# Tap softmax of a fused attention and mixture-of-experts kernel: two parts or three

## The reference, cut to what matters

```
# attention: x (2, 3584, 192), weight_gen (2, 3584, 8 heads, 7 taps), fp32
w = weight_gen - max(weight_gen, axis=-1)          # the tap softmax
w = exp(w);  w = w / (sum(w, axis=-1) + 1e-9)
x_pad = [6 zero rows, x]                            # per batch
out[s, h, :] = sum_k w[s, h, k] * x_pad[s + k, h, :]   # head h: 24 columns
# then mixture 1: noisy gate (x @ w_gate, softplus(x @ w_noise) * noise),
#   the best two of 8 experts, relu(x @ w1[e]) @ w2[e], weighted
# then mixture 2: gate by cosine to 8 embeddings, the best expert alone
```

## Time and profile before

| what | value |
| --- | --- |
| median of 3 runs | 1272.02 us (1271.82 to 1272.87) |
| the profiled execution's own time | 1273.49 us |
| its span | 1271.7 us |
| PE busy in the span | 1100.1 us (87%) |
| DVE busy | 791.9 us (62%) |
| POOL busy | 578.8 us (46%) |
| ACT busy | 552.8 us (43%) |
| first tap product starts | 20.75 us |
| product of the last group starts | 108.50 us |

### The profile page before, as it was taken

The page is one execution under the profiler, slowest core; times in us unless marked ns, Lnnn a source line. Parts: engine busy times, 40 slices in busy tenths (PEclk is TensorE's granted clock), DMA queues, the critical chain, the costliest instruction groups (busy, mean ns, idle before and its releaser), DMA issues.

```text
span 1271.7 us, 28030 instructions
## 1 busy us (share of the span) xinstructions
PE 1100.1 (87%) x7950; PEld 1024.6 (81%) x7951; DVE 791.9 (62%) x1447; ACT 552.8 (43%) x1544; POOL 578.8 (46%) x676
## 2 busy tenths in 40 slices
PE   1999045899999999999999999877179999999997
PEld 1566012799999999999999999856059999999997
DVE  8997899445555464645545464466964655466663
ACT  2112165445444454545444454346544544455552
POOL 5778065344444444444444444400544444444444
PEclk9999555899999999999999999988569999999999
DMA  9111200311313131221313111173603313114421
GB/s 319 70 51 62 58 0 0 90 39 42 97 38 93 43 98 37 62 70 41 101 37 89 43 39 40 37 239 110 232 19 95 94 41 96 42 50 131 130 57 36
DMA packets 51158, 97.51 MB, mean 77 GB/s; under 512 B 9651, under 2 KB 33051, under 8 KB 50876
## 3 DMA queue, kind: packets, MB, share of 16 engines
q1 hardware_dynamic: 33084, 61.77, 15.9%
q0 software_dynamic: 18048, 35.42, 9.7%
HBM read 69.62 MB, written 29.10 MB: 78 GB/s over the span
## 4 chain that ended last, share of the span: by engine, by line
PE 74%; DVE 16%; issue 4%; POOL 2%; ACT 1%; DMA 1%; DVEq 1%; ACTq 0%; POOLq 0%; SPq 0%
PE banks L624 21%; PE banks L626 10%; PE banks L610 8%; PE banks L612 7%; PE banks L611 7%; PE banks L616 7%; PE banks L615 7%; DVE prods L874 3%; PE banks L536 2%; DVE lo_hot L974 2%; POOL prods L410 2%; PE banks L595 2%; PE banks L596 2%; DVE hi_eq L967 2%; PE banks L577 1%
## 5 line engine op out<-in xcount | busy, mean ns | idle before, releaser
L1040 DVE SCALAR_TENSOR_TENSOR h_lo<-banks,h_hi 128x256 fp32r<-128x256 f32 x736 | 312.1, 424 | 380.6 <-ACT h_hi L761 377.5
L761 ACT ACTIVATE h_hi<-banks 128x256 fp32r<-128x256 f32 x736 | 282.5, 384 | 462.4 <-PE banks L616 462.2
L624 PE MATMUL banks<-w_hl,h_hi 128*128 128x384 f32 x1472 | 468.6, 355 | 0.6 <-issue 0.6
L626 PE MATMUL banks<-w_hl,h_lo 128*128 128x192 f32 x1472 | 370.7, 252 | 0.0
L626 PEld LDWEIGHTS banks<-w_hl,h_lo 128*128 128x128 f32 x1472 | 279.1, 190 | 0.0
L624 PEld LDWEIGHTS banks<-w_hl,h_hi 128*128 128x128 f32 x1472 | 276.6, 188 | 1.2 <-issue 1.1
L435 POOL DMA_INDIRECT x_slots<-token_rows,gather_idx x192 | 194.2, 1011 | 105.3 <-POOL gather_idx L432 76.0
L610 PE MATMUL banks<-x_hi_a,w_hi 128*128 (+1 forms) x736 | 227.3, 309 | 8.7 <-DVE h_lo L1040 8.6
L611 PE MATMUL banks<-x_hi_a,w_lo 128*128 (+1 forms) x736 | 207.3, 282 | 0.0
L612 PE MATMUL banks<-x_lo_a,w_hi 128*128 (+1 forms) x736 | 206.8, 281 | 0.0
L615 PE MATMUL banks<-x_hl_b,w_hi 128*128 (+1 forms) x736 | 206.0, 280 | 0.0
(11 more groups left out here) (174 smaller groups left out, 1424.9 us busy)
## 6 DMA issues: line engine op xcount, KB each, us to landing
raw<-in_moe_w SPq DMA_DIRECT2D x17, 768.0 KB
choices<-choice_rows SPq DMA_DIRECT2D x28, 384.0 KB, 3.8
raw<-in_moe_w SPq DMA_DIRECT2D x17, 512.0 KB
raw<-in_moe_w SPq DMA_DIRECT2D x34, 256.0 KB
x_halo<-in_x SPq DMA_DIRECT2D x2, 2688.0 KB, 15.4
token_rows<-stage SPq DMA_DIRECT2D x14, 384.0 KB, 2.3
token_rows<-rows SPq DMA_DIRECT2D x14, 384.0 KB, 4.0
x_slots<-token_rows,gather_idx POOLq DMA_INDIRECT x192
```

The lines of the kernel that those rows point to most:

```text
L624: mm(y[:, i, 0:2 * D], h_hi[:, c % HBUFS, t], w2_hl[u][:, c, :, :], start=c == 0, stop=False)
L626: ins = mm(y[:, i, 0:D], h_lo[:, c % HBUFS, t], w2_hl[u][:, c, 0, :], start=False, stop=c == FC - 1)
L761: sc.activation(h_hi[:, c % HBUFS, :], banks[:, c % HBANKS, 0:BLOCK], ACT.Relu).then_inc(h_hi_ready[m], 1)
L1040: v.scalar_tensor_tensor(h_lo[:, c % HBUFS, :], banks[:, c % HBANKS, 0:BLOCK], 0.0, h_hi[:, c % HBUFS, :].bitcast(F32), ALU.max, ALU.subtr ...
```

## The change

The softmax is done in three parts in place of two: part 0 is the first 8 rows of each partition in batch 0 (groups 0 and 1, 448 weights to a partition), part 1 the other 20 rows of batch 0 (groups 2 to 6, 1120 weights), part 2 batch 1 (groups 7 to 13, 1568 weights). SP loads weights and rows part by part, each row load after its own weights, and `emb` after all of them. DVE does subtraction and multiplication of part 0, POOL those of parts 1 and 2. The steps of parts 1 and 2 stand inside the group loop. The core of the diff:

```
+    PARTS = ((0, 0, 2 * GROUP), (0, 2 * GROUP, J), (1, 0, J))
...
@@ SP
+            load_weights(0)
+            load_x(0)          # two halo DMAs, then the rows
+            load_weights(1)
+            load_x(1)          # rows alone
+            load_weights(2)
+            load_x(2)          # two halo DMAs, then the rows
             sp.dma_start(emb_sb[0:E], emb).then_inc(emb_in, 16)
...
@@ POOL
+            def center(i):
+                pool.wait_ge(tap_max, i + 1)
+                gp.tensor_tensor(w, w, red.unsqueeze(2).to_broadcast(w.shape), ALU.subtract).then_inc(centered[i], 1)
+            def scale(i):
+                pool.wait_ge(exps, i + 1)
+                pool.wait_ge(tap_scale, i + 1)
+                gp.tensor_tensor(w, w, total.unsqueeze(2).to_broadcast(w.shape), ALU.mult).then_inc(weights_scaled[i], 1)
+            center(1)
             for g in range(NG):
                 ... three pair additions of group g ...
+                if g == 0:
+                    scale(1)
+                if g == 1:
+                    center(2)
+                if g == 4:
+                    scale(2)
...
@@ ACT
-            for b in range(B):
-                act.wait_ge(centered[b], 1)
-                sc.activation(attn_w[:, b], attn_w[:, b], ACT.Exp).then_inc(exps, 1)
-            act.wait_ge(emb_in, 16)
-            ... Square and sqrt of emb ...
+            exp_weights(0)
             take_weights(0)
             take_weights(1)
+            exp_weights(1)
             take_weights(2)
             take_turned(0, 0)
             for g in range(2, NG):
+                if g == 3:
+                    exp_weights(2)
                 if g + 1 < NG:
                     take_weights(g + 1)
                 take_logits(0, g - 2, 2 * E)
                 take_turned(0, g - 1)
+                if g == 4:
+                    ... wait for emb, Square and sqrt of emb ...
...
@@ DVE
+            taps_max(0)
+            ... subtraction of part 0 ...
+            taps_sum(0)        # sum, + 1e-9, reciprocal
+            ... multiplication of part 0 ...
             for g in range(NG):
+                for i in part_first(g):
+                    dve.wait_ge(x_in[i], 48 if PARTS[i][1] == 0 else 16)
                 ...
                 tap_products(g, 0, FIRST, first_prods)
+                if g == 0:
+                    taps_max(1)
                 tap_products(g, FIRST, SECOND, second_prods)
+                if g == 0:
+                    taps_sum(1)
+                if g == 1:
+                    taps_max(2)
+                if g == 3:
+                    taps_sum(2)
                 if g > 0:
                     dve.wait_ge(second_prods, g)
                     finish_rows(g - 1)
```

More of the change, by code:

```diff
@@ L178, in attention_moe_moe @@
         consts_ready = sem("consts_ready")
-        attn_w_in = [sem(f"attn_w_in{b}") for b in range(B)]
+        attn_w_in = [sem(f"attn_w_in{i}") for i in range(len(PARTS))]
         emb_in = sem("emb_in")
-        x_in = [sem(f"x_in{b}") for b in range(B)]
+        x_in = [sem(f"x_in{i}") for i in range(len(PARTS))]
         halo_zeroed = sem("halo_zeroed")
@@ L190, in attention_moe_moe @@
         emb_ready = sem("emb_ready")
-        centered = [sem(f"centered{b}") for b in range(B)]
+        centered = [sem(f"centered{i}") for i in range(len(PARTS))]
         tap_max = sem("tap_max")
         tap_scale = sem("tap_scale")
-        weights_scaled = [sem(f"weights_scaled{b}") for b in range(B)]
+        weights_scaled = [sem(f"weights_scaled{i}") for i in range(len(PARTS))]
         exps = sem("exps")
@@ L274, in turned_bank, with part_first, weight_part @@
             return 4 - 2 * u * m
+        def part_first(g):
+            b, jj = divmod(g, GB)
+            return [i for i, (at, lo, _) in enumerate(PARTS) if (at, lo) == (b, jj * GROUP)]
+        def weight_part(i):
+            b, lo, hi = PARTS[i]
+            heads = slice(lo * H, hi * H)
+            return attn_w[:, b, heads, :], attn_red[:, b, heads], tap_sum[:, b, heads]
         def logits_bank(m):
@@ L312, in _, with load_weights, load_x @@
             xt = x.rearrange("b (p j) d -> b p j d", p=P)
-            for b in range(B):
-                sp.dma_start(attn_w[:, b], weight_gen[b].rearrange("(p j) h k -> p (j h) k", p=P)).then_inc(attn_w_in[b], 16)
+            def load_weights(i):
+                b, lo, hi = PARTS[i]
+                rows = weight_gen[b].rearrange("(p j) h k -> p (j h) k", p=P)
+                sp.dma_start(weight_part(i)[0], rows[:, lo * H:hi * H, :]).then_inc(attn_w_in[i], 16)
+            def load_x(i):
+                b, lo, hi = PARTS[i]
+                if lo == 0:
+                    for first, end in ((1, 16), (16, P)):
+                        sp.dma_start(x_halo[first:end, b, 0:PAD], xt[b, first - 1:end - 1, J - PAD:, :]).then_inc(x_in[i], 16)
+                sp.dma_start(x_halo[:, b, PAD + lo:PAD + hi], xt[b, :, lo:hi, :]).then_inc(x_in[i], 16)
+            load_weights(0)
[4 more added lines that the diff above has]
+            load_x(2)
             sp.dma_start(emb_sb[0:E], emb).then_inc(emb_in, 16)
[L316 to L319, removed]
             for k, w in enumerate((m_gate, m_noise)):
@@ L693, in take_weights @@
                 b, jj = divmod(g, GB)
[L694 to L695 removed]
+                for i in part_first(g):
+                    act.wait_ge(weights_scaled[i], 1)
                 if g >= 2:
@@ L699, in take_weights, with exp_weights @@
                         attn_w[:, b, jj * GROUP * H:(jj + 1) * GROUP * H, :].rearrange("p a k -> p (a k)")).then_inc(w_in_psum, 1)
-            for b in range(B):
-                act.wait_ge(centered[b], 1)
-                sc.activation(attn_w[:, b], attn_w[:, b], ACT.Exp).then_inc(exps, 1)
-            act.wait_ge(emb_in, 16)
-            sc.activation(emb_sq[0:E], emb_sb[0:E], ACT.Square, accum_out=emb_norm[0:E, 0:1]).then_inc(act_step, 1)
-            act.wait_ge(act_step, 1)
-            sc.sqrt(emb_norm[0:E, 1:2], emb_norm[0:E, 0:1]).then_inc(emb_sumsq, 1)
+            def exp_weights(i):
+                w, _, _ = weight_part(i)
+                act.wait_ge(centered[i], 1)
+                sc.activation(w, w, ACT.Exp).then_inc(exps, 1)
+            exp_weights(0)
             take_weights(0)
             take_weights(1)
+            exp_weights(1)
             take_weights(2)
@@ L720, in _ @@
                 take_turned(0, g - 1)
+                if g == 4:
+                    act.wait_ge(emb_in, 16)
+                    sc.activation(emb_sq[0:E], emb_sb[0:E], ACT.Square, accum_out=emb_norm[0:E, 0:1]).then_inc(act_step, 1)
+                    act.wait_ge(act_step, 1)
+                    sc.sqrt(emb_norm[0:E, 1:2], emb_norm[0:E, 0:1]).then_inc(emb_sumsq, 1)
             take_logits(0, NG - 2, 2 * E)
@@ L848, in _, with taps_max, taps_sum @@
                 v.memset(t[DB:P, :, 0:width], 0.0)
[L850 to L865, removed]
+            def taps_max(i):
+                w, red, _ = weight_part(i)
+                dve.wait_ge(attn_w_in[i], 16)
+                v.tensor_reduce(red, w, AX.X, ALU.max).then_inc(tap_max, 1)
+            def taps_sum(i):
+                w, _, total = weight_part(i)
+                dve.wait_ge(exps, i + 1)
+                step(v.tensor_reduce(total, w, AX.X, ALU.add))
+                step(v.tensor_scalar(total, total, 1e-9, None, ALU.add))
+                v.reciprocal(total, total).then_inc(tap_scale, 1)
+            w, red, total = weight_part(0)
+            taps_max(0)
+            dve.wait_ge(tap_max, 1)
+            v.tensor_tensor(w, w, red.unsqueeze(2).to_broadcast(w.shape), ALU.subtract).then_inc(centered[0], 1)
+            taps_sum(0)
+            dve.wait_ge(tap_scale, 1)
+            v.tensor_tensor(w, w, total.unsqueeze(2).to_broadcast(w.shape), ALU.mult).then_inc(weights_scaled[0], 1)
             dve.wait_ge(halo_zeroed, B)
@@ L886, in _ @@
             for g in range(NG):
-                if g % GB == 0:
-                    dve.wait_ge(x_in[g // GB], 48)
+                for i in part_first(g):
+                    dve.wait_ge(x_in[i], 48 if PARTS[i][1] == 0 else 16)
                 dve.wait_ge(w_in_psum, g + 1)
```

10 lines of the change are left out of this document (2 added, 8 removed).

## The result

| | before | changed | forecast |
| --- | --- | --- | --- |
| median, us | 1272.87 (10 runs, 1271.82 to 1273.98) | 1276.36 (10 runs, 1274.39 to 1277.45) | 1276.0 (1271.5 to 1280.5) |
| ratio | 1 | 1.0025 (95% interval 1.0017 to 1.0034) | 1.0031 |
| span of the profiled execution | 1271.7 | 1275.0 | 1275.7 |
| first product | 20.75 | 8.24 | 8.5 |
| group 2's product | 33.50 | 28.24 | 28.5 to 29.5 |

The account below looks back on a forecast made before the run. The prediction took DVE to bound the loop, so moved-in work is paid there: -12.25 + 5.95 + 1.75 + 5.45 + 3.1 = +4.0 us, or 1276.0 us against the runs shown, range 1271.5 to 1280.5.

Parts of the forecast that it names:

- The start: Prologue: smaller part-0 weights land at 3.95, the part-0 chain takes 4.5, first product at 8.5; gain 12.25 us.
- Groups 0 and 1: Moved-in DVE work: part 1's softmax steps and waits in group 0, +5.95 us; part 2's maximum in group 1, +1.75.
- The wait for Exp: Group 0: DVE waits 0.95 us for POOL's subtraction and ACT's Exp of part 1, beyond its second product's cover.
- the adding: Group 0: DVE's addition of 1e-9 to part 1's 160 sums, blocked by POOL's additions, taken as 1.2 us.
- Group 3: Part 2's Exp wait of 1.7 us, sum 1.79, adding 0.3, reciprocal 1.55 and hand-overs 0.1 on DVE: +5.45 us.
- rival 2: PE falls to 1.2 GHz already ahead of group 2, and again later: +5.5 to +9 us, time 1279.5; chance 0.15.
- Group 4: Through ACT, +3.1 us: `emb` work makes group 6's weights 1.5 late, PE's low clock adds 1.4 to 1.6.
- the list order: ACT's `emb` work, 2.13 us, stands ahead of group 6's weights with 0.6 of slack: 1.5 us late.
- Groups 6 to 13: Rest of the loop: each group runs at 6.82 us, and what follows the loop keeps its length.
- Rival 1: Work comes without small waits: PE's clock holds, adding unblocked, or weights sooner; +0.5 to +2.5 us, time 1273.5; chance 0.24.
- Rival 3: DVE never waits in groups 0 to 6, only its own work is left: -2.8 us, time 1269.2; chance 0.07.
- Rival 4: Group 0: POOL blocks the adding through all three additions, to 20.7, costing 1.7 more: 1277.7; chance inside the forecast's 0.54.

Follow-up runs that it names:

- all_aside: Changed kernel, part 2's Exp and `emb` work moved into ACT's idle time, part 1's sum later, no 1e-9 addition, unread matmuls added: 1269.28 us, ratio 0.9971.
- no_eps: Changed kernel without the addition of 1e-9 in its three parts: 1275.73 us, 1.0028 of the kernel before.
- clock_fill: Changed kernel with unread matmuls added in PE's idle stretches ahead of the pair sums of groups 2 and 4: 1273.64 us, 1.0008 of the kernel before.
- exp_aside: Changed kernel with ACT's Exp of part 2 moved to iteration 2, behind the weights of group 3: 1274.83 us, 1.0015 of the kernel before.
- no_part2: Changed kernel without the softmax of batch 1, whose raw weights are multiplied: 1265.69 us, 0.9944 of the kernel before.
- emb_aside: Changed kernel with ACT's `emb` work moved ahead of iteration 4's logits copy, where ACT is idle: 1273.43 us, 1.0009 of the kernel before.
- shift_48: Kernel before with three idle DVE reductions (4.9 us) ahead of its first product: 1277.40 us, 1.0040 of the kernel before.
- late_sum: Changed kernel with part 1's sum, addition and reciprocal moved behind group 1's first product: 1277.01 us, 1.0034 of the kernel before.
- shift_24: Kernel before with two idle DVE reductions (1.8 + 0.6 us) ahead of its first product: 1275.41 us, 1.0026 of the kernel before.

## Why the prediction was right

The forecast was +4.0 us, measured +3.5 in the median (1.0025, or 2.2 to 4.3 us by its interval) and +4.8 at the loop's end. By its own steps, each from product start to product start:

- **The start**, forecast 12.25: 12.51. The weights landed at 3.7, as reckoned (3.95). The rows of part 0 were the weak place: in this execution the copy of the weights released the first product, but in eight of the nine experiments that share this start it was the rows' DMA, with waits of 0.55 to 1.81 us and starts from 8.15 to 9.04. The forecast had said that they come "just ahead" and that a delay is added in full; against the changed kernel it was up to 0.8 us (all_aside).
- **Groups 0 and 1**, forecast 5.95 + 1.75 = 7.70: 7.25 (group 2's product 20.00 after the first, 12.75 before). The wait for Exp was 0.97 (forecast 0.95), the adding 1.08 (1.2). no_eps took 1.12 out by leaving it away.
- **Group 3**, forecast 5.45: 6.76. This is the term that was mis-sized. The wait on Exp was 3.12 and not 1.7, because PE's clock fell behind the idle stretch ahead of group 2 (four matmuls took 2.93 us). The forecast put nothing for it, though it had that stretch at up to 2.9 us and one of 2.48 had cost the clock in the earlier trace rows; rival 2 named it. clock_fill kept the clock up and the wait was 1.60; exp_aside took it out altogether. Whether every execution of the changed kernel has this fall is not shown: after the same idle time exp_aside's trace has none.
- **Group 4**, forecast 3.1: 3.28, of it 2.59 a wait on ACT's copy and 0.73 one ahead of finish 4, for PE's slow sums. With the clock kept up, 1.29 is left in clock_fill and 1.28 in no_part2: that is the list order, forecast 1.5. The clock's part is then 1.99, forecast 1.6. emb_aside, without the list order, is left with 1.04. Each part alone costs less than its share of the 3.28, because ACT's slack takes up some of it. The forecast also called as a witness of the low clock; in the trace of the kernel before the granted clock reads 1.00 over these 12 matmuls (26 to 33 us), so that row does not show it, and the earlier trace rows do.
- **Groups 6 to 13** at 6.82, as forecast (113.29 - 65.55 is seven times 6.82). Group 4's product came 1.5 later than before, not 0.9, and nothing was in hand any more.

Together -12.51 + 7.25 + 6.76 + 3.28 = +4.78 at group 6. That the median came out under the forecast is partly luck: 0.8 us more loss in the loop than forecast, and about 1.3 less of it in the median. For the single profiled pair the granted clock at the two mixtures' starts goes with the 1.5 us; why the changed kernel's median lies at 3.5 where shift_48, with 0.6 us less at the loop's end, lies at 4.7 is open, and the intervals (2.2 to 4.3 and 3.4 to 6.9 us) overlap.

The rivals: rival 2's mechanism came, a fall ahead of group 2 worth about 1.4, but not its +5.5 to +9, because the start and groups 0 and 1 came out 0.7 better than the forecast's terms and the later fall added 2.0, not 3. Rival 1 did not come: the clock fell and the adding met POOL. Rival 3's condition, no wait between DVE's instructions up to group 6, does not hold in the changed kernel; all_aside builds it, and being also without the adding it lies 3.7 us under the kernel before where rival 3, with it, had 2.8. Rival 4 is wrong: in group 0 the adding ended at 18.70, while POOL's three additions ran from 15.01 to 20.36. DVE came in between two of them.

## What to carry to other kernels

In a loop bound by one engine, taking that engine's work out of the prologue and putting it between the iterations gains only the idle time it fills and the steps that leave the engine; price the move as the start's gain less every moved instruction, and then look for the waits. A step that fits easily into an engine's mean idle time can still sit in front of the one instruction that has no slack: place it by that engine's list, ahead of the long wait and not behind it. A gain ahead of a wait that another chain ends is worth nothing (late_sum), and idle time handed to TensorE can come back as a lower clock on the next group's sums.

## What the runs showed of the hardware

- In the changed kernel PE idle for 1.77 us ahead of group 1 kept its clock, idle for 2.82 ahead of group 2 lost it, and the fall did not come at once: the first four matmuls after the stretch took 1.53 us, the next four 2.93. The length of the stretch alone does not decide: 2.53 lost the clock in no_eps (and in late_sum ahead of group 2), while 2.84 in exp_aside and 2.90 in late_sum ahead of group 1 kept it. The 4.5 us ahead of group 4 lost it in each of the six traces that have them. The stretch of 2.90:

```profile
25.90 1.56 PE L568 MATMUL banks<-prods,ident 128*128 128x384 f32 x4 [2.90 <-POOL prods L436]
27.68 1.56 PE L568 MATMUL banks<-prods,ident 128*128 128x384 f32 x4 [0.22 <-POOL prods L436]
```

- A DVE addition of a constant, 0.28 us undisturbed for 224 numbers, took 1.08 (160 numbers), 1.38 and 1.83 us beside POOL's additions of 1.8 each. The last two ended 0.13 us after POOL's third addition; DVE's reductions, reciprocals and products beside the same additions kept their durations (1.78, 1.55, 3.35).
- Behind the loop single executions of kernels that are the same there differ by almost 4 us: the shift of the loop's end less that of the span was 2.9 in emb_aside, 2.1 in shift_24, 0.5 in shift_48 and -1.0 in exp_aside.
